# Where the second experts' row gathers stand in GpSimd's queue

## The chip, the cores and the metric

The kernel runs on one core of one Trainium2 chip. The metric is the device time of one execution in microseconds (us). The core has five engines with a queue of instructions each: TensorE (PE, with its weight loads shown apart as PEld), VectorE (DVE), ScalarE (ACT), GpSimd (POOL) and SyncE (SP). They meet only at semaphores. An engine whose next instruction waits holds up everything that is queued behind it on the same engine. Transfers run on 16 DMA engines, which serve the queues of all issuers.

## What is computed

A gated scan over 4 sequences of 5056 tokens with 256 features gives 20224 rows. These pass through a first layer of 8 experts with a fixed capacity, and then through a second layer of 8 experts, in which each row goes to the expert with the highest logit. The change touches the second layer only:

```python
logits = x @ w_gate                       # x: 20224 x 256, 8 experts
expert_idx = np.argmax(logits, axis=1)
...
for e in range(E):
    mask = expert_idx == e
    xe = x[mask]
    h = np.maximum(xe @ w1[e], 0.0)       # 256 -> 1024
    ye = h @ w2[e]                        # 1024 -> 256
    out[mask] = gate_w[mask, None] * ye
```

How many rows an expert has is known only on the chip.

## The kernel before

`scan_stage`, `route_and_experts` and `experts_top1` run one behind the other. The last of them, from about 1409 us to 2404 us of the trace, is the second layer.

**Blocks.** Rows are worked in blocks of 256, as two tiles of 128. In the profiled execution there are 83 blocks: experts 0 to 7 have 11, 7, 10, 10, 13, 13, 7 and 12 of them. The loops over an expert's blocks take their limits from `plan`, a tile in on-chip memory. Block `i` (from 0) uses the columns `i` of `rows_i` (row numbers) and `skip`.

**TensorE** (`compute(i, b)`, L1819). For each of 8 slices of 128 hidden features there is an `up` (L1804: six matmuls, 3 terms by 2 halves of the input) and a `down` (L1815: six matmuls). The `down`s follow three slices behind. After the last `up`, TensorE waits until the rows of block `i + 1` have been gathered into `xg` (L1826), transposes them (L1794, four 128x128 transposes) and then does the last three `down`s. So the transposes of block `i + 1` stand some 2.5 us ahead of the end of block `i`. There is one buffer `xg`.

**ScalarE and VectorE** turn each slice into a high part `hh` (L1851) and a low part `hl` (L1891). After the transposes ScalarE copies the last two columns of each row of `xg` to `meta` (L1855; this counts `meta_kept`). At the end of a block they scale the result by the gate: tile 0 on ScalarE (L1867), tile 1 on VectorE (L1905). These write `rows`, of which there is one buffer, once `rows_free` has been counted.

**GpSimd** has three kinds of work here, all in one queue:

- `gather(i)` (L1734 to L1745) waits until block `i - 1` has been transposed and its `meta` kept, copies two columns of row numbers to `idx` (L1739), and issues two indirect DMAs that fill `xg` with the rows of block `i` (L1743).
- `scatter_before(i)` (L1747) waits for the rows of block `i - 1` and issues two indirect DMAs that write them to the output (L1754).
- `split_up` and `split_down` (L557, L564) make the high and the low part of the next expert's two weight matrices, four casts (L549) and four subtractions (L553) each. They are done for experts 1 to 7, so in the parts of experts 0 to 6.

Turn `i` of GpSimd is `pass_on(i)`: wait until the scatter of the turn before has landed, count `rows_free`, gather block `i + 1`, scatter block `i - 1`. The turns of an expert are `first + 1` to `end`. Around the first of them stand the splits: `split_up`, turn `first + 1`, `split_down`, then the loop (L1783) over the other turns. Here `first` is the expert's first block.

**SyncE** loads the raw weights of the expert after the next (L542, L543: 1 MB each) as soon as `split_down` is done. There are seven pairs of loads (experts 1 to 7). The first stands at the beginning of the stage, and six follow a `split_down`, those in the parts of experts 0 to 5.

Of the kernel before, what the change touches and what calls it, by code (L numbers as in the profile page):

```python
# [49 lines left out]
T2 = C2 // P  # L50
# [63 lines left out]
def alone(eng, passed):  # L114

    eng.sem_inc(passed, 1)
# [440 lines left out]
def split_up(pool, c, b, split, before):  # L557

    half = F // 2
    here = [(slice(None), d, slice(q * half, (q + 1) * half)) for d in range(DH) for q in range(2)]  # L560
    split_pieces(pool, [(c.w1_raw[at], c.w1_s[b][0][at], c.w1_s[b][1][at]) for at in here], split, before)


def split_down(pool, c, b, split, before, scores=True):  # L564

    here = [(slice(None), slice(g, g + 2), slice(0, D)) for g in range(0, FC, 2)]
    split_pieces(pool, [(c.w2_raw[at], c.w2_s[b][0][at], c.w2_s[b][1][at]) for at in here], split, before)
    if scores:
        at = (slice(None), slice(None), slice(D, D + E))
        split_pieces(pool, [(c.w2g[:], c.w2_s[b][0][at], c.w2_s[b][1][at])], split, before + 2)  # L570
# [1104 lines left out]
def experts_top1(nc, c, src, w1, w2, dst):  # L1675
# [3 lines left out]
    with ExitStack() as ctx:  # L1679
# [20 lines left out]
        gathered = c.xg2_gathered  # L1700
# [16 lines left out]
        def all_blocks(eng):  # L1717
            return eng.value_load(c.plan[0:1, E - 1:E], min_val=E, max_val=B2)

        def blocks_of(eng, e):  # L1720

            end = eng.value_load(c.plan[0:1, bass.ds(e, 1)], min_val=1, max_val=B2)
            first = eng.value_load(c.plan[0:1, bass.ds(E + e, 1)], min_val=0, max_val=B2 - 1)
            return first, end

        @block.sync
        def _(sp):
            with sp.Fori(1, E) as e:
                sp.wait_ge(split, 4 * e)
                load_weights(sp, c, w1, w2, e, raw)  # L1730

        @block.gpsimd
        def _(pool):
            def gather(i):  # L1734
                pool.wait_ge(x_turned, DH * i)
                pool.wait_ge(meta_kept, i)
                pool.wait_ge(gathered, 16 * T2 * i)
                alone(pool, passed)
                pool.tensor_copy(idx[:], c.rows_i[:, bass.ds(i * T2, T2)]).then_inc(idx_ready, 1)  # L1739
                pool.wait_ge(idx_ready, i)  # L1740
                alone(pool, passed)
                for k in range(T2):
                    pool.indirect_dma_start(xg[:, k, :].bitcast(I32), None, src[:, :],  # L1743
                                            bass.IndirectOffsetOnAxis(ap=idx[:, k:k + 1].bitcast(U32), axis=0)
                                            ).then_inc(gathered, 16)  # L1745

            def scatter_before(i):  # L1747

                pool.wait_ge(rows_a, i + 1)
                pool.wait_ge(rows_b, i + 1)  # L1750
                pool.wait_ge(dest_ready, i)
                alone(pool, passed)
                for k in range(T2):
                    pool.indirect_dma_start(dst[:, :], bass.IndirectOffsetOnAxis(ap=dest[:, k:k + 1].bitcast(U32), axis=0),  # L1754
                                            rows[:, k, :], None, bounds_check=N - 1, oob_is_err=False
                                            ).then_inc(scattered, 16)

            def pass_on(i, first=False):

                if not first:  # L1760
                    pool.wait_ge(scattered, 16 * T2 * (i - 1))
                pool.sem_inc(rows_free, 1)
                gather(i + 1)
                scatter_before(i)

            pool.sem_inc(split, 4)
            gather(1)
            for e in range(E):
                first, end = blocks_of(pool, e)

                if e + 1 < E:
                    pool.wait_ge(raw, 32 * (e + 1))
                    if e > 0:
                        pool.wait_ge(h_used, FC * first + AHEAD)
                        alone(pool, passed)
                    split_up(pool, c, (e + 1) % 2, split, 4 * (e + 1))
                pass_on(first + 1, first=e == 0)
                if e + 1 < E:
                    split_down(pool, c, (e + 1) % 2, split, 4 * (e + 1) + 2, scores=False)
                second = pool.snap(first + 2, min_val=2, max_val=B2)  # L1780
                after = pool.snap(end + 1, min_val=2, max_val=B2 + 1)
                with pool.If(after > second):
                    with pool.Fori(second, after) as i:  # L1783
                        pass_on(i)
            total_blocks = all_blocks(pool)
            pool.wait_ge(gathered, 16 * T2 * (total_blocks + 2))
            pool.wait_ge(scattered, 16 * T2 * total_blocks)

        @block.tensor
# [165 lines left out]
```

## Time and profile before

| | us |
|---|---|
| median of 3 runs | 2413.83 (2413.49 to 2415.52) |
| the profiled execution, its own time | 2420.34 |
| its span in the trace | 2418.6 |
| PE busy, in the span | 2275.1 (94%) |
| POOL busy, in the span | 954.6 (39%) |
| second experts, first matmul to last | 1411.73 to about 2403.8 |

The span is what the trace covers. The 1.7 us beside it lie before and behind, and a run without the profiler was some 6.5 us shorter. TensorE is busy nearly all of the second experts' stage. GpSimd's busy time is its instructions on the engine: for an indirect DMA that is the time in which it is issued, and the data move later. "Idle before" in a row of the timeline is the time since the engine's last instruction, and behind the arrow stands what ended it.

### The profile page before, as it was taken

To read this page: it belongs to the slowest core of one execution; us is meant where nothing else is said; L and a number is where in the kernel's file an instruction comes from. 1 tells how busy PE (TensorE), PEld (TensorE's weight loads), DVE (VectorE), ACT (ScalarE), POOL (GpSimd) and SP (SyncE) were. 2 spreads that over 40 slices of the span, in tenths; PEclk is the share of its full clock that TensorE was granted. 3 is DMA by queue.
4 is the path that set the end of the run, shared out by engine and by line. 5 is a ranking of instruction groups with operands and counts; after the bars stand their busy time and mean duration, and the time that the engine had idled before them with its cause. 6 is when DMAs were issued, how large, how long until landed. Compare 5 with 4: busy or idle time off the path is not lost. (4 is left out here: it accounts for less than half of the span.)

```text
span 2418.6 us, 51799 instructions
## 1 busy us (share of the span) xinstructions
PE 2275.1 (94%) x18040; PEld 2115.4 (87%) x18041; DVE 1385.8 (57%) x3385; ACT 809.9 (33%) x2027; POOL 954.6 (39%) x1035
## 2 busy tenths in 40 slices
PE   7883699999999999999999869999999999999997
PEld 7882588888888888888898869999999999999997
DVE  8887876776767777676644443333333333333332
ACT  4440324242332423223333223333333333333332
POOL 5660133333333333333433353535353535335333
PEclk9996699999999999999999979999999999999998
DMA  7894112121211212121221131122121212111111
GB/s 271 286 318 154 53 36 71 40 68 43 71 36 40 73 39 70 44 71 36 77 75 42 45 104 46 40 82 77 43 75 47 78 44 68 53 44 42 41 45 39
DMA packets 86191, 182.95 MB, mean 76 GB/s; under 512 B 14318, under 2 KB 50929, under 8 KB 86066
## 3 DMA queue, kind: packets, MB, share of 16 engines
q0 software_dynamic: 31872, 85.58, 11.5%
q1 hardware_dynamic: 40722, 82.34, 9.9%
q10 hardware_dynamic: 13472, 13.37, 2.0%
q8 instruction: 77, 1.26, 0.2%
q14 instruction: 48, 0.39, 0.1%
HBM read 118.94 MB, written 64.13 MB: 76 GB/s over the span
## 5 line engine op out<-in xcount | busy, mean ns | idle before, releaser
L1891 DVE SCALAR_TENSOR_TENSOR m_hl<-m_hP,m_hh 128x256 fp32r<-128x256 f32 x664 | 275.0, 424 | 538.3 <-ACT m_hh L1851 486.4
L1851 ACT ACTIVATE m_hh<-m_hP 128x256 fp32r<-128x256 f32 x664 | 247.6, 384 | 516.9 <-PE m_hP L1804 516.2
L1111 ACT ACTIVATE m_hh<-m_hP 128x512 fp32r<-128x512 f32 (+1 forms) x320 | 189.9, 593 | 630.3 <-PE m_hP L976 624.6
L837 POOL DMA_INDIRECT y_rows<-spare,m_dest x164 | 180.9, 1103 | 537.9 <-DVE m_dest L1454 489.3
L1414 DVE SCALAR_TENSOR_TENSOR m_hl<-m_hP,m_hh 128x512 fp32r<-128x512 f32 (+1 forms) x320 | 218.6, 683 | 274.9 <-ACT m_hh L1111 253.2
L827 POOL DMA_INDIRECT spare<-h_rows,m_idx x164 | 193.9, 1182 | 57.1 <-issue 37.5
L1743 POOL DMA_INDIRECT xg<-y_rows,m_idx x168 | 166.0, 988 | 96.1 <-POOL m_idx L1739 70.5
L1754 POOL DMA_INDIRECT out_dram<-m_rows,m_dest x166 | 168.2, 1013 | 54.5 <-issue 54.5
L1739 POOL COPY m_idx<-rows_i 128x2 int32 (+1 forms) x84 | 15.5, 184 | 398.7 <-ACT m_meta L1855 380.9
L1804 PE MATMUL m_hP<-xh,w_0h 128*128 128x256 f32 x656 | 131.8, 282 | 11.2 <-issue 11.2
L1815 PE MATMUL m_yP<-w_1h,m_hh 128*128 128x256 f32 x672 | 139.2, 289 | 1.0 <-DVE m_hl L1891 1.0
L1804 PE MATMUL m_hP<-xh,w_1h 128*128 128x256 f32 x672 | 134.2, 281 | 2.1 <-issue 2.1
L1815 PE MATMUL m_yP<-w_0h,m_hh 128*128 128x256 f32 x656 | 136.1, 289 | 0.0
L1815 PE MATMUL m_yP<-w_1h,m_hl 128*128 128x256 f32 x672 | 134.1, 281 | 0.0
L1815 PE MATMUL m_yP<-w_1l,m_hh 128*128 128x256 f32 x672 | 133.7, 280 | 0.0
L1804 PE MATMUL m_hP<-xh,w_1l 128*128 128x256 f32 x672 | 133.3, 280 | 0.0
L1804 PE MATMUL m_hP<-xl,w_1h 128*128 128x256 f32 x672 | 133.3, 279 | 0.0
L1815 PE MATMUL m_yP<-w_0h,m_hl 128*128 128x256 f32 x656 | 131.1, 281 | 0.0
L1804 PE MATMUL m_hP<-xh,w_0l 128*128 128x256 f32 x656 | 130.9, 281 | 0.0
L1804 PE MATMUL m_hP<-xl,w_0h 128*128 128x256 f32 x656 | 130.8, 281 | 0.0
L1815 PE MATMUL m_yP<-w_0l,m_hh 128*128 128x256 f32 x656 | 130.6, 280 | 0.0
L986 PE MATMUL m_yP<-w_0h,m_hh 128*128 128x264 f32 x640 | 114.0, 300 | 4.4 <-DVE m_hl L1414 2.3
(306 smaller groups left out, 5708.7 us busy)
## 6 DMA issues: line engine op xcount, KB each, us to landing
spare<-in_moe_w_dram SPq DMA_DIRECT2D x32, 1024.0 KB, 5.6
f_in<-in_f_logit_dram SPq DMA_DIRECT2D x39, 512.0 KB, 4.5
x_in<-in_x_dram SPq DMA_DIRECT2D x39, 512.0 KB, 5.3
h_rows<-rows ACTq DMA_DIRECT2D x25, 512.0 KB, 4.5
h_rows<-spare SPq DMA_DIRECT2D x14, 512.0 KB, 6.2
xg<-y_rows,m_idx POOLq DMA_INDIRECT x168
out_dram<-m_rows,m_dest POOLq DMA_INDIRECT x166
spare<-h_rows,m_idx POOLq DMA_INDIRECT x164
```

Of the source, the lines that this page charges most:

```text
L827: pool.indirect_dma_start(xg[:, k, :], None, src[:, :], bass.IndirectOffsetOnAxis(ap=idx[:, k:k + 1].bitcast(U32), axis=0)).then_inc(gathe ...
L837: pool.indirect_dma_start(dst[:, :], bass.IndirectOffsetOnAxis(ap=dest[:, k:k + 1].bitcast(U32), axis=0), rows[(i - 1) % 2][:, k, 0:ROW].b ...
L986: mm = pe.matmul(yP[:, k, 0:WIDE], h[f % 2][:, k * P:(k + 1) * P], c.w2_s[b][s][:, f, 0:WIDE], start=(f == 0 and q == 0), stop=(f == FC - ...
L1111: act.activation(hh[f % 2][:, tokens(i)], hP[f % 2][:, tokens(i)], ACT.Relu).then_inc(hh_ready, 1)
L1414: dve.scalar_tensor_tensor(out=hl[f % 2][:, tokens(i)], in0=hP[f % 2][:, tokens(i)], scalar=0.0, in1=hh[f % 2][:, tokens(i)].bitcast(F32), ...
L1739: pool.tensor_copy(idx[:], c.rows_i[:, bass.ds(i * T2, T2)]).then_inc(idx_ready, 1)
L1743: pool.indirect_dma_start(xg[:, k, :].bitcast(I32), None, src[:, :], bass.IndirectOffsetOnAxis(ap=idx[:, k:k + 1].bitcast(U32), axis=0)).t ...
L1754: pool.indirect_dma_start(dst[:, :], bass.IndirectOffsetOnAxis(ap=dest[:, k:k + 1].bitcast(U32), axis=0), rows[:, k, :], None, bounds_chec ...
L1804: mm = pe.matmul(hP[f % AHEAD], c.w1_s[b][s][:, d, f * P:(f + 1) * P], x[:, d, :], start=(q == 0), stop=(q == len(terms) - 1))
L1815: mm = pe.matmul(yP[k], h[f % AHEAD][:, k * P:(k + 1) * P], c.w2_s[b][s][:, f, 0:D], start=(f == 0 and q == 0), stop=(f == FC - 1 and q == 2))
L1851: act.activation(hh[f % AHEAD][:], hP[f % AHEAD], ACT.Relu).then_inc(hh_ready, 1)
L1891: dve.scalar_tensor_tensor(out=hl[f % AHEAD][:], in0=hP[f % AHEAD], scalar=0.0, in1=hh[f % AHEAD][:].bitcast(F32), op0=ALU.max, op1=ALU.su ...
```

## The change

`gather(i + 1)` leaves `pass_on`. `gather(i)` now stands directly in front of `pass_on(i)` in the loop. For the first turn of each expert but expert 0 it stands ahead of `split_up`; for expert 0 that is the `gather(1)` that was there before. There is no gather of the block behind the block behind the last any more, and the wait at the end counts one gather less.

```diff
@@ -1760,7 +1760,6 @@
                 if not first:
                     pool.wait_ge(scattered, 16 * T2 * (i - 1))
                 pool.sem_inc(rows_free, 1)
-                gather(i + 1)
                 scatter_before(i)
 
             pool.sem_inc(split, 4)
@@ -1768,6 +1767,8 @@
             for e in range(E):
                 first, end = blocks_of(pool, e)
 
+                if e > 0:
+                    gather(first + 1)
                 if e + 1 < E:
                     pool.wait_ge(raw, 32 * (e + 1))
                     if e > 0:
@@ -1781,9 +1782,10 @@
                 after = pool.snap(end + 1, min_val=2, max_val=B2 + 1)
                 with pool.If(after > second):
                     with pool.Fori(second, after) as i:
+                        gather(i)
                         pass_on(i)
             total_blocks = all_blocks(pool)
-            pool.wait_ge(gathered, 16 * T2 * (total_blocks + 2))
+            pool.wait_ge(gathered, 16 * T2 * (total_blocks + 1))
             pool.wait_ge(scattered, 16 * T2 * total_blocks)
```

GpSimd's queue at an expert with splits, from the subtractions of `split_up` to those of `split_down`. `w_0h` and `w_0l` are the parts of the weights (the first pair those of w1, the second those of w2), `xg` is what a gather fills, `out_dram` what a scatter writes:

```order
 L553 TENSOR_TENSOR w_0l<-spare,w_0h 128x512 x4
 L1761 REGISTER_ALU
-L1735 ISA
-L1737 REGISTER_ALU
-L1739 ISA
-L1739 COPY m_idx<-rows_i 128x2
-L1743 DMA xg<-y_rows,m_idx 128x258 x2
-L1751 REGISTER_ALU
+L1749 REGISTER_ALU
 L1754 DMA out_dram<-m_rows,m_dest 20224x256 x2
 L549 CAST w_0h<-spare 128x2x256 x4
 L553 TENSOR_TENSOR w_0l<-spare,w_0h 128x2x256 x4
```

The gather between the two splits is gone. It was the gather of block `first + 2`.

GpSimd's loop over an expert's other turns, before:

```order
190 L1783 ISA
191 L1735 ISA
192 L1737 REGISTER_ALU
193 L1739 ISA
194 L1739 COPY m_idx<-rows_i 128x2
195 L1743 DMA xg<-y_rows,m_idx 128x258 x2
196 L1754 DMA out_dram<-m_rows,m_dest 20224x256 x2
```

and the same loop in the changed kernel, with the two splits' last instruction in front of it:

```order
182 L553 TENSOR_TENSOR w_1l<-spare,w_1h 128x2x256 x4
183 L1783 REGISTER_ALU
184 L1783 COMPARE_AND_BRANCH
185 L1784 UNCONDITIONAL_BRANCH
186 L1784 ISA
187 L1737 REGISTER_ALU
188 L1739 ISA
189 L1739 COPY m_idx<-rows_i 128x2
190 L1743 DMA xg<-y_rows,m_idx 128x258 x2
191 L1761 ISA
192 L1749 REGISTER_ALU
193 L1754 DMA out_dram<-m_rows,m_dest 20224x256 x2
```

The loop holds the same copy and the same four DMAs in the same order, but the gather in it is that of the turn's own block, one block earlier in the count. The first gather of the loop, that of block `first + 2`, now stands behind `split_down`. The orders of TensorE and SyncE are the same in both kernels.

## Rows read from the trace of the kernel before

**Rows 1.** Waits of 1380 to 2418 us: us in total, times, longest

```profile
PE m_tP L1794 <- DMA xg<-y_rows,m_idx: 3.0, 2, 2.1
```

**Rows 2.** Timeline of one ordinary turn: start us, us, engine, line, what

```profile
1506.69 0.46 PEld L1794 LDWEIGHTS m_tP<-ident,xg 128*128 128x128 f32 x4
...
1507.84 0.18 POOL L1739 COPY m_idx<-rows_i 128x2 int32 x1 [5.82 <-ACT m_meta L1855]
...
1508.86 1.01 POOL L1743 DMA_INDIRECT xg<-y_rows,m_idx  x1 [0.83 <-POOL m_idx L1739]
...
1509.58 0.48 DVE L1905 TENSOR_SCALAR m_rows<-m_yP,m_gate 128x256 f32<-128x256 f32 x1 [0.99 <-PE m_yP L1815]
...
1510.17 0.97 POOL L1743 DMA_INDIRECT xg<-y_rows,m_idx  x1 [0.30 <-DVE m_rows L1905]
...
1511.45 1.01 POOL L1754 DMA_INDIRECT out_dram<-m_rows,m_dest  x1 [0.30 <-issue]
...
1512.77 1.01 POOL L1754 DMA_INDIRECT out_dram<-m_rows,m_dest  x1 [0.30 <-issue]
...
1518.45 0.46 PEld L1794 LDWEIGHTS m_tP<-ident,xg 128*128 128x128 f32 x4
```

**Rows 3.** Timeline of the first experts: a scatter's DMA behind the wait it had

```profile
723.25 0.16 DVE L1454 TENSOR_TENSOR m_dest<-m_dest_f,m_skip 128x4 int32<-128x4 f32 x1
...
724.32 1.01 POOL L837 DMA_INDIRECT y_rows<-spare,m_dest  x1 [11.66 <-DVE m_dest L1454]
```

**Rows 4.** Timeline: block 0's gather, alone, and the transposes that waited for it

```profile
1399.12 1.18 POOL L858 DMA_INDIRECT xg<-y_rows,rows_i  x1 [0.30 <-issue]
...
1402.13 0.29 PEld L1077 LDWEIGHTS m_tP<-ident,xg 128*128 128x128 f32 x2 [14.19 <-issue]
```

**Rows 5.** Timeline of POOL around the start of expert 1

```profile
1549.04 2.30 POOL L549 CAST w_0h<-spare 128x512 fp32r<-128x512 f32 x4
1551.42 5.04 POOL L553 TENSOR_TENSOR w_0l<-spare,w_0h 128x512 fp32r<-128x512 f32 x4
1556.41 0.18 POOL L1739 COPY m_idx<-rows_i 128x2 int32 x1
...
1558.73 0.96 POOL L1743 DMA_INDIRECT xg<-y_rows,m_idx  x1 [0.31 <-DVE m_rows L1905]
```

**Rows 6.** Timeline of PE around the same start: transposes of blocks 11, 12 and 13

```profile
1542.07 0.60 PE L1794 MATMUL m_tP<-ident,xg 128*128 128x128 f32 x4
1545.35 0.50 PE L1804 MATMUL m_hP<-xh,w_1h 128*128 128x256 f32 x2 [0.55 <-issue]
...
1555.16 0.60 PE L1794 MATMUL m_tP<-ident,xg 128*128 128x128 f32 x4
1567.07 0.60 PE L1794 MATMUL m_tP<-ident,xg 128*128 128x128 f32 x4
```

**Rows 7.** Timeline: two gathers beside a weight load, and the transposes that waited

```profile
1439.25 0.37 SPq L542 DMA_DIRECT2D spare<-in_moe_w_dram  x1
...
1441.37 0.96 POOL L1743 DMA_INDIRECT xg<-y_rows,m_idx  x1 [0.30 <-issue]
...
1447.83 0.66 PE L1794 MATMUL m_tP<-ident,xg 128*128 128x128 f32 x4 [0.88 <-DMA xg<-y_rows,m_idx]
...
1777.47 0.96 POOL L1743 DMA_INDIRECT xg<-y_rows,m_idx  x1 [0.30 <-issue]
...
1783.48 0.66 PE L1794 MATMUL m_tP<-ident,xg 128*128 128x128 f32 x4 [2.12 <-DMA xg<-y_rows,m_idx]
```

**Rows 8.** Timeline of PE: block 0 of the stage, from its first matmul

```profile
1411.73 0.79 PE L1804 MATMUL m_hP<-xh,w_0h 128*128 128x256 f32 x2 [8.48 <-issue]
...
1423.09 0.60 PE L1794 MATMUL m_tP<-ident,xg 128*128 128x128 f32 x4
```

**Rows 9.** Stretches: us, busy of PE, PEld, DVE, ACT, POOL, granted clock, DMA share, GB/s

```profile
1416.00:1416.50 0.50, 0.50 (x4) 0.50 (x4) 0.11 (x1) 0.36 (x1) 0.00 (x0) 0.58 1.01 326
...
2406.00:2406.50 0.50, 0.00 (x0) 0.00 (x0) 0.00 (x0) 0.00 (x0) 0.50 (x1) 0.79 0.35 91
```

## The prediction

> **What bounds the kernel now.** I read the summary by engine first (TensorE busy 94% of the span), then the waits, then the timelines of an ordinary turn and of an expert's start. From 1411.7 to 2403.8 us the second experts are a row of TensorE blocks, one every 11.76 us (the two weight loads of the transposes in [rows 2]). GpSimd is not what TensorE waits for: for a gather TensorE waited twice, 3.0 us in all [rows 1]. The reader is to see the reason in [rows 2]: the gather goes out as soon as the single buffer `xg` is free (1507.84), its second DMA starts at 1510.17, and the transposes that need it come at 1518.45. That is 8.28 us from the DMA's start to the need. The change gives this slack away, since each gather now goes behind the scatter of the block before. So the question is how long a gather needs from the moment at which the rows of a finished block are ready.
>
> **Ordinary turns.** After the change GpSimd waits for `rows`, scatters, then gathers for the transposes that end the running block. The chain is, from one start of the transposes:
> - 3.37 us until `rows` is ready (1506.69 to 1509.58 + 0.48) [rows 2]
> - 0.91 us from the semaphore to the first scatter DMA. This wait is not in the second stage, where the scatter always stands behind a running gather; the nearest row is the first experts' scatter, 723.41 to 724.32 [rows 3]
> - 1.32 us to the second scatter DMA, 1.01 us for it, 1.02 us from the copy of the indices to the first gather DMA, 1.31 us to the second [rows 2]
> - from its start to the data: 3.01 us in [rows 4], where the DMA itself took 1.18 instead of 0.97 us; I take 2.80.
>
> Together 11.74 us against 11.76 us. The wait for the former scatter, which now stands behind the gather, costs nothing: that scatter was issued two DMAs earlier, and `rows` is wanted only at the end of the block. So ordinary turns are level to a few hundredths, and I can't say from the rows on which side. Of the 82 gathers that the change moves (blocks 2 to 83, with 83 read by no `up`), 7 are the late ones of the next part and 7 stand ahead of a split or at the start of expert 7, where TensorE itself loses time between experts (13.09 us between the transposes at 1542.07 and 1555.16 [rows 6]), so 68 remain. I take 0.05 us each, 3.4 us, with the bounds 0 (every link 0.1 shorter) and 0.3 each, 20 us.
>
> **The first turns of experts 0 to 6.** Here is the main cost. The gather of block `first + 2` stood between the two splits and now stands behind `split_down`. A split takes 7.42 us (1549.04 to 1556.46 [rows 5]); `split_down` has as many casts and subtractions of the same size, and I take the same for it. For expert 1:
> - transposes of block `first` at 1542.0, `rows` ready at 1545.3, scatter DMAs at 1546.2 and 1547.5, copy of indices 1548.5, gather of `first + 1` at 1549.5 and 1550.9. It lands at 1553.7, ahead of the transposes at 1555.1 [rows 6]: no wait.
> - `split_up` 1551.8 to 1559.2. It is now behind that gather. The rows of block `first` are ready at 1555.1 + 3.4 = 1558.5, so the scatter is not held by them and follows at 1559.5 and 1560.9.
> - `split_down` 1561.8 to 1569.2, the copy at 1569.2, the gather DMAs at 1570.3 and 1571.6. Before, the second one was at 1558.73 [rows 5].
> - Alone it lands 2.80 us later, at 1574.4, against transposes that were due at 1567.0 [rows 6]: TensorE waits 7.4 us.
> - It is not alone. SyncE loads 2 MB of weights as soon as `split_down` ends. In the kernel before, the loop's first gather met the same load in the same order, the load 2.1 us ahead of the second gather DMA: 1439.25 and 1441.37, and the transposes could start only at 1447.8 [rows 7]. That is 6.4 us from the DMA's start instead of 2.8. At the other late gather it was 5.9 us (1777.47 to 1783.4 [rows 7]). I take 6.15, between them. The wait is then 10.7 us.
>
> The six loads that follow a `split_down` belong to experts 0 to 5, expert 6 has none behind it. Expert 0's first part begins with weights that come late, but its two splits and gathers stand in the same row; I count it the same. So 6 x 10.7 + 7.4 = 71.6 us. The gathers that waited before, 0.88 and 2.12 us [rows 7], now follow a long stop and a full block, so their 3.0 us go: net 68.6 us. Bounds: with no collision 6 x 3.3 = 20 us less; with 6.4 us in each 1.5 us more.
>
> The Trainium skill has a rule against this collision: by "DMA: Bandwidth & Descriptors", section "Queues, rings and completion order", each DMA engine takes turns between the queues that have work, packet by packet. By that rule a gather of a few packets an engine would hardly notice the load, and the sum would be 20 us less. [Rows 7] speak against it, with 6.4 us.
>
> **TensorE's clock.** The granted clock was at the lower of its two levels (0.50, 1.2 GHz) while the stage began, and rose to 2.4 GHz at about 1416.4 us [rows 9], 4.7 us after the first matmul at 1411.73 [rows 8]. At the end of the kernel it fell some 2.5 us after TensorE stopped (0.79 in the half microsecond from 2406.0) [rows 9]. All seven waits of this forecast are longer than that, so each should be followed by slow matmuls. Price: 4.7 us at half speed lose 2.35 us; block 0 took 11.36 us from its first matmul to the transposes [rows 8], another expert's first block 9.81 us (1545.35 to 1555.16 [rows 6]), which is 1.55 us. I take 2.1 between them: 7 x 2.1 = 14.7 us, bounds 0 and 16.5 us. These blocks give GpSimd more time, so no further gather is late for it.
>
> **The rest.** The last turn no longer issues a gather ahead of its scatter. Before, the first scatter DMA came 1.39 us behind `rows` (1510.06 to 1511.45 [rows 2]); now 0.91. That is 0.5 us off the end. One gather less moves 264 KB less, hidden. The last expert has no splits, so its first turns are ordinary.
>
> **Sum.** 68.6 + 14.7 + 3.4 - 0.5 = 86.2 us on the profiled execution, whose own time is 2420.34: 2506.5. The median of the runs shown is 2413.83, 6.5 us below that execution; the added waits don't depend on this, so the forecast is 2413.8 + 86.2 = 2500 us, 3.6% slower.
>
> **Rivals.**
> - *The gather beside the weight load lands as if alone.* The time is 20 us less: 2480. For it: only two such gathers were seen waiting. Against it: both were late. The rule of the Trainium skill named above ("DMA: Bandwidth & Descriptors") would give this one. Chance 0.13.
> - *Ordinary turns are late too.* If the chain is 12.0 to 12.2 us instead of 11.74, TensorE waits in each of 68 turns and the period of the stage becomes the chain: 14 to 31 us more beyond my 3.4 at most, 2511 to 2528. For it: the sum has no slack, and its two uncertain links (0.91 and 2.80) come from other stages. Chance 0.17.
> - *The clock doesn't fall.* 14.7 us less, 2486. For it: the rows show the clock fall only once TensorE has stopped for good. Against it: that fall came sooner after the stop than any of the seven waits would end. Chance 0.06.
> - *Not slower.* GpSimd would issue the gather's DMAs while its casts and subtractions run, so that `split_down` holds up nothing. Then the seven waits are not there, and the 3.0 and 0.5 us are gained: 2410, within 0.2% of before. It decides from the point at which the gather of `first + 2` starts its second DMA by 1567.0 - 2.8 = 1564.2 instead of 1571.6. Against it: the copy of the indices behind a split starts where the split ends (1556.41 [rows 5]), though nothing held it back, and a scatter's DMA starts 0.30 us behind a gather's [rows 2]. Chance 0.04.
> - The forecast as summed: chance 0.60, own range 2490 to 2512.
>
> **Numbers.** The range 2474 to 2522 takes in the forecast, the clock and the collision rivals and half of the late ordinary turns. A measurement of this kernel can tell about 0.2% (4.8 us) from no change. Slower by over 0.2%: 0.96. Within 0.2%: 0.03, nearly all of the last rival. Faster by over 0.2%: 0.01.
>
> **What would show it.** In the changed kernel the waits of the transposes (L1794) for the gather should be about 75 us, in seven waits of 7 to 11 us, one an expert but the last, the one without a weight load the shortest; ahead of each, on GpSimd, two splits with only a scatter between them. Behind each the granted clock should be 0.50 for 4 to 5 us. In ordinary turns the second gather DMA should start some 2.8 us ahead of the transposes, and the period be 11.8. If the period is 12 or more, the second rival holds. If the seven waits are all near 7.4 us, the first does. If there are none, my reading of GpSimd's queue is wrong.

## The result, and the profile after

| | before | after |
|---|---|---|
| median of 5 runs, us | 2413.49 (2412.79 to 2415.52) | 2506.16 (2504.57 to 2508.11) |
| ratio to before, with its 95% interval | | 1.0383 (1.0371 to 1.0395) |
| the profiled execution, its own time | 2420.34 | 2504.57 |
| its span | 2418.6 | 2502.8 |

The change costs 92.7 us. The forecast was 2500 in a range of 2474 to 2522.

The page of after, its parts 1 and 5 (in the last: what is done, how often, busy us and mean ns, then the idle time before it and what ended that):

```profile
PE 2283.4 (91%) x18040; PEld 2123.6 (85%) x18041; DVE 1390.1 (56%) x3385; ACT 820.0 (33%) x2027; POOL 953.0 (38%) x1032
...
L1796 PE MATMUL m_tP<-ident,xg 128*128 128x128 f32 x332 | 54.7, 290 | 79.8 <-DMA xg<-y_rows,m_idx 79.7
```

TensorE does the same work (18040 matmuls in both; 2275.1 us busy before, 2283.4 now, and the 8 us more fit the stretches at the lower clock further down), but 79.7 us of idle time stand in front of the transposes, and a gather ended them. The lines have moved: what was L1794 is L1796, L1905 is L1907. The waits of 1380 to 2503 us (in total, times, longest) answer to [rows 1], where it was 3.0 us in two waits:

```profile
POOL out_dram L1754 <- DVE m_rows L1907: 503.0, 76, 11.8
...
PEld m_tP L1796 <- DMA xg<-y_rows,m_idx: 83.4, 18, 12.2
...
PE m_tP L1796 <- DMA xg<-y_rows,m_idx: 79.7, 15, 12.0
```

The first line is the new wait of GpSimd, in nearly every turn: it now stands in front of the scatter, with the gather queued behind it. That costs nothing by itself. An ordinary turn of after, answering to [rows 2]:

```profile
1507.05 0.48 DVE L1907 TENSOR_SCALAR m_rows<-m_yP,m_gate 128x256 f32<-128x256 f32 x1 [0.99 <-PE m_yP L1817]
...
1508.46 1.01 POOL L1754 DMA_INDIRECT out_dram<-m_rows,m_dest  x1 [6.10 <-DVE m_rows L1907]
1509.77 0.99 POOL L1754 DMA_INDIRECT out_dram<-m_rows,m_dest  x1 [0.30 <-issue]
...
1511.80 1.01 POOL L1743 DMA_INDIRECT xg<-y_rows,m_idx  x1 [0.83 <-POOL m_idx L1739]
...
1513.12 0.96 POOL L1743 DMA_INDIRECT xg<-y_rows,m_idx  x1 [0.30 <-issue]
...
1515.90 0.46 PEld L1796 LDWEIGHTS m_tP<-ident,xg 128*128 128x128 f32 x4
```

The reader is to see that the last line has no bracket, so TensorE didn't wait, and that the second gather DMA starts 2.78 us ahead of it instead of 8.28. The slack is spent. From `rows` ready (1507.53) to the scatter's DMA are 0.93 us.

GpSimd at the start of expert 1, answering to [rows 5], with the weight load of SyncE (`SPq`) and the transposes of block `first + 2`:

```profile
1564.15 5.02 POOL L553 TENSOR_TENSOR w_0l<-spare,w_0h 128x512 fp32r<-128x512 f32 x4
...
1569.33 1.02 POOL L1754 DMA_INDIRECT out_dram<-m_rows,m_dest  x1 [0.17 <-issue]
...
1570.66 1.01 POOL L1754 DMA_INDIRECT out_dram<-m_rows,m_dest  x1 [0.31 <-issue]
...
1571.65 2.30 POOL L549 CAST w_0h<-spare 128x512 fp32r<-128x512 f32 x4
...
1574.03 4.98 POOL L553 TENSOR_TENSOR w_0l<-spare,w_0h 128x512 fp32r<-128x512 f32 x4
...
1578.97 0.17 POOL L1739 COPY m_idx<-rows_i 128x2 int32 x1
...
1579.18 0.37 SPq L542 DMA_DIRECT2D spare<-in_moe_w_dram  x1
...
1581.30 0.96 POOL L1743 DMA_INDIRECT xg<-y_rows,m_idx  x1 [0.30 <-issue]
...
1587.32 1.12 PE L1796 MATMUL m_tP<-ident,xg 128*128 128x128 f32 x4 [10.90 <-DMA xg<-y_rows,m_idx]
```

Between the two splits is only a scatter. The gather goes out behind `split_down`, in step with the load, and the transposes start 6.0 us after its second DMA. Stretches around that wait (us, busy time of PE, PEld, DVE, ACT and POOL, granted clock, DMA share, GB/s):

```profile
1576.00:1581.00 5.00, 0.42 (x4) 0.22 (x2) 0.42 (x1) 0.38 (x1) 4.14 (x5) 1.00 0.13 19
...
1582.00:1587.00 5.00, 0.00 (x0) 0.00 (x0) 0.00 (x0) 0.00 (x0) 0.26 (x1) 0.50 1.04 373
...
1587.00:1587.50 0.50, 0.18 (x1) 0.18 (x2) 0.00 (x0) 0.11 (x1) 0.00 (x0) 0.50 0.26 78
...
1588.00:1591.00 3.00, 3.00 (x16) 3.00 (x15) 0.92 (x3) 0.74 (x2) 0.00 (x0) 0.50 0.03 5
...
1592.00:1593.00 1.00, 1.00 (x11) 1.00 (x10) 0.48 (x1) 0.68 (x2) 0.00 (x0) 1.00 0.00 0
```

TensorE stops at 1576.4. The clock is still full up to 1581 and falls behind that, during the stop. It stays at its lower level of 1.2 GHz for some 4 us of work behind it (16 matmuls in 3 us, later 11 in one), and comes back at 1591 to 1592. The DMA engines are full until 1587.1, and the transposes start 0.2 us later: the gather was there about when the last of the load was.

**Where the time is.** I took the distance from one block's transposes to the next one's, for all 82 pairs of both traces, by the start of the transposes' weight loads, and grouped them by the block that the later transposes are for (an expert's blocks counted from `first`):

| distances ending at | before | after | difference |
|---|---|---|---|
| block `first + 2`, 7 of them | 83.28 | 157.53 | +74.25 |
| block `first + 3`, 7 | 86.53 | 94.83 | +8.30 |
| block `first + 1` of experts 1 to 7, 7 | 90.44 | 89.85 | -0.59 |
| the other 61 | 717.69 | 723.02 | +5.33 |
| sum | 977.94 | 1065.23 | +87.3 |

The table gives 87.3 us and the medians 92.7. The stage began 2.4 us earlier in after's profiled execution (1409.31 instead of 1411.73) and ended 0.7 us earlier behind its last rows, so that the two profiled executions differ by 84.2 us. The one of before was 6.9 us above the median of its runs, that of after 1.6 us below its own. In which stage before's profiled execution spent those 6.9 us the record doesn't show, so the place of what the table leaves open isn't known either. The profiler by itself doesn't make an execution so much longer: the profiled executions of the other kernels are 1.6 us below to 4.5 us above their medians. Beside the experiments below the kernel before had medians of 2414.78, 2419.72 and 2419.29 us, on three chips. On the second of these a repeat of after cost 88.8 us (ratio 1.0362), and the distances in its trace sum to 1068.4 us.

### The profile page after: what moved, and what is told of

Read it like the earlier page. It is cut to its first block and busy times, and to the rows that moved or that the text cites. A ratio compares the mean times of both kernels' runs of the same rounds, so it can differ in the third digit from the quotient of the medians.

```text
span 2502.8 us, 51866 instructions
## 1 busy us (share of the span) xinstructions
PE 2283.4 (91%) x18040; PEld 2123.6 (85%) x18041; DVE 1390.1 (56%) x3385; ACT 820.0 (33%) x2027; POOL 953.0 (38%) x1032
## 3 DMA queue, kind: packets, MB, share of 16 engines
q0 software_dynamic: 31776, 85.32, 10.9%
## 5 line engine op out<-in xcount | busy, mean ns | idle before, releaser
L1893 DVE SCALAR_TENSOR_TENSOR m_hl<-m_hP,m_hh 128x256 fp32r<-128x256 f32 x664 | 282.1, 425 | 524.4 <-ACT m_hh L1853 524.4
L1853 ACT ACTIVATE m_hh<-m_hP 128x256 fp32r<-128x256 f32 x664 | 254.8, 384 | 502.4 <-PE m_hP L1806 502.4
L1806 PE MATMUL m_hP<-xh,w_0h 128*128 128x256 f32 x656 | 131.8, 282 | 11.3 <-issue 11.3
L1796 PE MATMUL m_tP<-ident,xg 128*128 128x128 f32 x332 | 54.7, 290 | 79.8 <-DMA xg<-y_rows,m_idx 79.7
```

What stands on the lines that cost most here:

```text
L1796: t = pe.transpose(tP[d][:, k * P:(k + 1) * P], xg[:, k, d * P:(d + 1) * P], c.ident[:])
L1806: mm = pe.matmul(hP[f % AHEAD], c.w1_s[b][s][:, d, f * P:(f + 1) * P], x[:, d, :], start=(q == 0), stop=(q == len(terms) - 1))
L1853: act.activation(hh[f % AHEAD][:], hP[f % AHEAD], ACT.Relu).then_inc(hh_ready, 1)
L1893: dve.scalar_tensor_tensor(out=hl[f % AHEAD][:], in0=hP[f % AHEAD], scalar=0.0, in1=hh[f % AHEAD][:].bitcast(F32), op0=ALU.max, op1=ALU.su ...
```

## The experiments

**My theory.** Three things make up the change's cost: the seven gathers that now stand behind `split_down`, the clock that falls while TensorE waits for them, and a landing that the weight load puts off. **The rivals**: that ordinary turns cost a good part of it (the chain through the scatter has no slack), that the load only happens to be beside the gather, and that the clock is a sign and no cost. Experts here have at least 7 blocks, which the edits make use of. Each experiment was run beside the kernel before. The ratios below are to it.

### One part alone: only the first turns

The kernel before, with only the gather of block `first + 2` moved behind `split_down`. Ordinary turns stay as they were.

```diff
-                gather(i + 1)
+                if ahead:
+                    gather(i + 1)
                 scatter_before(i)
...
-                pass_on(first + 1, first=e == 0)
+                pass_on(first + 1, first=e == 0, ahead=e + 1 == E)
                 if e + 1 < E:
                     split_down(pool, c, (e + 1) % 2, split, 4 * (e + 1) + 2, scores=False)
+                    gather(first + 2)
```

> The kernel before, but for experts 0 to 6 the gather of block first + 2 is moved behind split_down; all other gathers stay ahead of the scatter of the turn before theirs. Theory: seven waits of 7 to 12 us and seven slow blocks come with it, the short waits of ordinary turns don't: 2413.5 + 73.7 - 3.0 + 12.8 = 2497, within 2492 to 2501. Rival, that the long waits need the later gathers in front of them as well (the gather of first + 1, and split_up behind it): the waits are shorter by the 2.3 us by which split_up starts sooner, 7 x 2.3 = 16 us less, 2481.

Measured: 2494.20 us (2493.43 to 2498.54), ratio 1.0326 (1.0309 to 1.0343), 79.4 us over before. Its waits:

```profile
PEld m_tP L1796 <- DMA xg<-y_rows,m_idx: 73.4, 7, 11.1
```

They are seven: six of 10.9 to 11.1 us and one of 7.3. The short waits of after are absent. The distances to `first + 2` and `first + 3` are 155.86 and 97.18 us, together 83.2 more than before, and the other 68 are 3.9 us shorter in all than before's, for which I have no reason. So 79 of the 93 us come with this one gather an expert. The move of the others is worth the rest, some 14 us by the ratios (their intervals leave it between 9 and 19), of which the two spans show 6 (2502.8 and 2496.8) and the distances 7.9 (1065.23 and 1057.32). Which is nearest I can't say.

### The load out of the way

After, but SyncE's load waits until the late gather has landed. GpSimd waits for that landing too, ahead of the turn's scatter.

```diff
                 sp.wait_ge(split, 4 * e)
+                sp.wait_ge(load_ok, e)
                 load_weights(sp, c, w1, w2, e, raw)
...
+                if e + 1 < E:
+                    gather(second)
+                    pool.wait_ge(gathered, 16 * T2 * (second + 1))
+                    pool.sem_inc(load_ok, 1)
+                    pass_on(second)
```

> The changed kernel, but SyncE's weight load that follows split_down waits in addition until the gather of block first + 2 has landed. Theory: the load is what makes six of the seven gathers land 3.3 us later than alone, so the six waits of 10.6 to 12.0 us become about 7.4 us like the seventh: 2506.2 - 6 x 3.4 = 2486, within 2482 to 2490. Rival, that the gathers are late by themselves and the load has no share: 2506. If the DMA engines took turns packet by packet between the two queues, as the rule of the Trainium skill says (DMA: Bandwidth & Descriptors, Queues, rings and completion order), the change would also be small.

Measured: 2485.20 us (2484.57 to 2485.65), ratio 1.0289 (1.0272 to 1.0306). The same place as above, in expert 1:

```profile
1579.07 0.96 POOL L1745 DMA_INDIRECT xg<-y_rows,m_idx  x1 [0.30 <-issue]
...
1581.81 1.12 PE L1805 MATMUL m_tP<-ident,xg 128*128 128x128 f32 x4 [7.71 <-DMA xg<-y_rows,m_idx]
1582.02 0.37 SPq L542 DMA_DIRECT2D spare<-in_moe_w_dram  x1
```

2.74 us from the DMA's start to the transposes instead of 6.02, and the load follows. All seven waits (of the weight loads) are 7.4 to 8.8 us. The distances to `first + 2` fall by 20.6 us (157.53 to 136.97), and nothing else changes by more than 0.7. The load costs six gathers 3.4 us each: it is the cause, and not merely beside them. After itself agrees. Its seventh late gather, of expert 6, has no load, and the transposes start 2.9 us after its second DMA, where the other six took 5.7 to 6.4 us.

### The clock kept up

After, with 84 matmuls into the transposes' PSUM tile ahead of the long wait. Nothing reads their result. They take most of the time of the wait.

```diff
...
+                if busy is not None:
+                    with pe.If(busy < E - 1):
+                        for _ in range(84):
+                            pe.matmul(tP[0], c.w1_s[b][0][:, 0, 0:P], xh[:, 0, :], start=True, stop=True)
                 pe.wait_ge(gathered, 16 * T2 * (i + 2))
...
```

> The changed kernel, but TensorE does 84 matmuls more, whose result nobody reads, ahead of its wait for the gather of block first + 2 in experts 0 to 6 (84 x 0.117 = 9.8 us). Theory: the slow blocks behind the long waits (12.8 us together beyond ordinary ones) come from the clock, which fell to 1.2 GHz while TensorE stood still; with TensorE busy it stays up, and the matmuls are hidden in the waits but for 2.4 us in expert 6, whose wait is 7.4 us: 2506.2 - 12.8 + 2.4 = 2496, within 2493 to 2499. Rival, that these blocks are slow for another reason (the chain through GpSimd): 2506.2 + 2.4 = 2509.

Measured: 2495.81 us (2493.89 to 2497.22), ratio 1.0331 (1.0314 to 1.0348). The 84 matmuls, the transposes behind them, and the stretch that follows:

```profile
1574.68 9.96 PE L1831 MATMUL m_tP<-xh,w_1h 128*128 128x256 f32 x84
...
1586.08 0.66 PE L1796 MATMUL m_tP<-ident,xg 128*128 128x128 f32 x4 [1.45 <-DMA xg<-y_rows,m_idx]
...
1586.00:1590.00 4.00, 3.92 (x34) 3.92 (x35) 1.31 (x4) 1.70 (x5) 0.00 (x0) 1.00 0.00 0
```

The gather is as late as in after, but the clock is 1.00 behind the wait, with 34 matmuls in 4 us. The distances to `first + 3` come to 83.54 us instead of 94.83. 11.3 us are the clock's. With useless work for TensorE the kernel is 10 us faster than with a wait (medians 2495.81 and 2506.16, though not run side by side). In the distances to `first + 2` the extra matmuls cost 3.9 us.

### The gather back between scatter and split

After, but the gather of `first + 2` goes out ahead of `split_down` again, as before.

```diff
                 if e + 1 < E:
+                    gather(first + 2)
                     split_down(pool, c, (e + 1) % 2, split, 4 * (e + 1) + 2, scores=False)
...
+                if e + 1 < E:
+                    pass_on(second)
```

> The changed kernel, but for experts 0 to 6 the gather of block first + 2 is put between the scatter of turn first + 1 and split_down, and the loop begins with that turn's scatter. All other gathers stay where the change put them. Theory of the forecast: the seven long waits (73.7 us in the changed kernel) and the slow clock behind each of them (7 blocks that took 12.8 us longer than ordinary ones) hang on split_down alone, so both go; the gather's second DMA starts about 2.8 us ahead of the need and no weight load is near it. 2506.2 - 73.7 - 12.8 = 2420, within 2416 to 2425. Rival, that each gather behind its scatter costs, in all turns: it stays above 2440.

Measured: 2452.86 us (2450.28 to 2453.70), ratio 1.0153 (1.0136 to 1.0170). I was wrong. The time is where my rival put it (above 2440), but its reason isn't the one, for the loss isn't in all turns. The transposes for `first + 2` hardly wait any more (four times, 0.2 to 1.1 us), but those for `first + 3` do:

```profile
1573.99 1.03 POOL L1754 DMA_INDIRECT out_dram<-m_rows,m_dest  x1
1574.01 0.37 SPq L542 DMA_DIRECT2D spare<-in_moe_w_dram  x1
...
1578.69 0.97 POOL L1743 DMA_INDIRECT xg<-y_rows,m_idx  x1 [0.30 <-issue]
...
1583.70 0.72 PEld L1800 LDWEIGHTS m_tP<-ident,xg 128*128 128x128 f32 x4 [3.65 <-DMA xg<-y_rows,m_idx]
```

`split_down` now holds up the scatter of the next turn, the gather of `first + 3` stands behind that scatter, and both meet the load. By distances: 85.88 us to `first + 2`, 105.91 to `first + 3`, 91.65 to `first + 4`. In the last the clock is at work, which had fallen in six waits of 3.4 to 3.6 us. The other distances are within 0.8 us of after's in all. What follows: the split isn't harmful only in front of the one gather. With no gather a block ahead, `split_down` makes one late at either of the two places tried. The distances to `first + 2`, `first + 3` and `first + 4` are together 82 us longer than before's where it stands ahead of the gather, and 31 us where it stands behind.

### Both: the gather back, and the load behind

The kernel above, and SyncE's load waits until the gather of `first + 3` has landed.

```diff
...
+                    with pool.Fori(third, fourth) as i:
+                        gather(i)
+                        pool.wait_ge(gathered, 16 * T2 * (i + 1))
+                        pool.sem_inc(load_ok, 1)
+                        pass_on(i)
...
```

> The kernel of the run early_again (gather of first + 2 ahead of split_down), but the weight load waits until the gather of block first + 3 has landed. In early_again that gather followed split_down and a scatter and was beside the load: its second DMA started at 1578.69 and the transposes came at 1583.70, 3.65 us after TensorE was ready. Theory: alone it lands 2.8 us after its start, at 1581.5, so the six waits are 1.4 instead of 3.6 to 3.8 us, too short for the clock to fall: 6 x 2.2 = 13 us less for the waits and 9 us less for the clock: 2452.9 - 22 = 2431, within 2425 to 2436. Rival, that the load has no share: 2453.

Measured: 2434.14 us (2433.71 to 2435.65), ratio 1.0056 (1.0041 to 1.0072). The distances to `first + 3` are 92.91 us instead of 105.91, those to `first + 4` 82.26 instead of 91.65. In the first of the two a wait is left:

```profile
1582.69 0.42 PEld L1810 LDWEIGHTS m_tP<-ident,xg 128*128 128x128 f32 x4 [1.47 <-DMA xg<-y_rows,m_idx]
```

Of the 93 us of the change all but 14 are gone. By distances 15 are left over before: 6.4 to `first + 3` (92.91 against 86.53), 2.7 to `first + 2`, and 6.8 in the 61 others, where after has 5.3. All gathers but the seven that went back still stand as in after.

### A longer step in every turn

After, with a fill of a 128x512 tile on GpSimd ahead of each gather of the loop. Nothing reads the tile. It is there to see how much slack ordinary turns have.

```diff
                     with pool.Fori(second, after) as i:
+                        pool.memset(step[:], 0.0)
                         gather(i)
```

> The changed kernel, with one more instruction of GpSimd (a fill of 128x512 numbers that nobody reads, an estimate of 0.3 to 0.6 us by the casts of that size, 0.58 us each) ahead of each gather of the loop. Theory: ordinary turns are level, so what a gather starts later TensorE waits longer: 68 turns x 0.3 to 0.6 = 20 to 41 us more than the changed kernel, and nearly every ordinary turn shows a wait. Rival, that ordinary turns still have slack of half a microsecond or more, since the profile shows only 8 short waits: less than 8 us more.

Measured: 2540.06 us (2539.13 to 2541.01), ratio 1.0497 (1.0481 to 1.0513). That is 31.6 us over a repeat of after (below), whose kernel before ran at 2419.72 on its chip, against 2419.29 here.

```profile
PEld m_tP L1798 <- DMA xg<-y_rows,m_idx: 120.1, 74, 12.5
...
1502.53 0.56 POOL L1786 MEMSET m_step<- 128x512 f32 x1
1503.00 0.21 POOL L1740 COPY m_idx<-rows_i 128x2 int32 x1
...
1520.33 0.42 PEld L1798 LDWEIGHTS m_tP<-ident,xg 128*128 128x128 f32 x4 [0.47 <-DMA xg<-y_rows,m_idx]
```

The copy starts 0.47 us later than in after, and the gather is waited for in nearly all turns (74 waits, 18 in after). The period is 12.1 to 12.2 us. In the 54 distances that end at neither `first + 1` nor `first + 2`, `+ 3` or `+ 4` the sum is 666.71 us where after has 640.72, 0.48 a turn. So all of the added 0.47 shows: ordinary turns of after have no slack that I can measure, and they lose nothing by it as long as nothing is added.

### The eight short waits

Beside the seven long waits after has eight of 0.3 to 1.7 us, 6.0 us in all, by the matmuls of the transposes. (Their weight loads show eleven, each 0.2 us longer; the three more are at last blocks of experts too.) Five of the eight are at the last block of an expert and one at the block behind the last of all. In these, places without a row all point at the same row of zeros (the last block of expert 7 has 27 rows for its 256 places). Two are elsewhere. The gather of expert 7's last block in after:

```profile
2469.53 0.97 POOL L1743 DMA_INDIRECT xg<-y_rows,m_idx  x1 [0.30 <-issue]
...
2473.14 0.42 PEld L1796 LDWEIGHTS m_tP<-ident,xg 128*128 128x128 f32 x4 [0.79 <-DMA xg<-y_rows,m_idx]
```

3.6 us from the second DMA to the transposes instead of 2.8. At the eight last blocks it is 3.0 to 3.3 us with fewer than 100 empty places (four blocks) and 3.6 to 3.7 us with more (four), and 3.8 at the block behind the last, in which all 256 are empty. The experiment keeps 128 rows of zeros, one for each partition, and lets the empty place in partition `p` read row `p` of them. The kernel is otherwise after.

```diff
-            sp.dma_start(dst[E * N:E * N + 1, :], zero[:]).then_inc(zero_stored, 16)
+            sp.dma_start(dst[E * N:E * N + P, :], zero[:]).then_inc(zero_stored, 16)
...
-                st.do(dve.tensor_scalar(c.rows_i[:, tiles], row_f[:, tiles], float(E * N), None, ALU.add))
+                st.do(dve.tensor_scalar(c.rows_i[:, tiles], row_f[:, tiles], pad[:], None, ALU.add))
```

> The changed kernel, but the empty places of a block don't all read the one zero row behind the data: place p reads a zero row p of its own (128 zero rows instead of one). The changed kernel's short waits for a gather (8 in all, 6.0 us) are, but for two, those of experts' last blocks and of the block behind the last, and in those rows most places are empty. Theory: many reads of one row make such a gather 0.6 to 1.0 us slower, and with its own rows each such wait goes: six waits, 3.5 us less, 2502.7 if the changed kernel is at 2506.2 on this chip. Rival, that these gathers are slow by chance or by the block's place: no change (within 1 us).

Measured: 2503.86 us (2503.20 to 2505.49), ratio 1.0346 (1.0332 to 1.0360). A repeat of after on the same chip:

> The changed kernel itself, beside the next ones on the same chip: 2506, within 2503 to 2509.

Measured: 2508.51 us (2506.82 to 2509.69), ratio 1.0362 (1.0348 to 1.0376). The own rows are 4.65 us faster, with ranges that don't meet. The waits of the repeat, then those of the experiment and its gather of the same block:

```profile
PEld m_tP L1796 <- DMA xg<-y_rows,m_idx: 85.3, 18, 12.2
```

```profile
PEld m_tP L1798 <- DMA xg<-y_rows,m_idx: 79.0, 9, 12.2
...
2482.34 0.96 POOL L1745 DMA_INDIRECT xg<-y_rows,m_idx  x1 [0.30 <-issue]
...
2485.17 0.42 PEld L1798 LDWEIGHTS m_tP<-ident,xg 128*128 128x128 f32 x4
```

2.83 us again, and no wait. All last blocks are at 2.8 to 2.9 us. The two waits that are not at last blocks are still there (1.13 and 1.88 us by the weight loads, 1.04 and 1.84 in after). These two gathers don't land late (2.8 us in after), they go out late. Between their two DMAs GpSimd stands still for 2.20 us instead of 0.30. The second of them in after, and what stands at the same place of the count before:

```profile
2164.43 0.96 POOL L1743 DMA_INDIRECT xg<-y_rows,m_idx  x1 [2.20 <-issue]
```

```profile
2089.22 1.01 POOL L1754 DMA_INDIRECT out_dram<-m_rows,m_dest  x1 [2.27 <-issue]
```

In all twelve traces it is the 444th and the 556th indirect DMA of GpSimd that come so late. In before both are a scatter's second DMA, and no transposes wait for such a scatter itself. (But the first of them stands ahead of expert 3's `split_up`, and expert 3 has the longer of the two waits of [rows 1], 2.12 us, where experts 1, 2, 4 and 5 have none.) After has two DMAs fewer ahead of each scatter, so the same place in the count falls on the second DMA of a gather without slack. What happens at that place the record doesn't show. Expert 3's long wait, 12.02 us where the other five with a load have 10.6 to 11.0, fits it too: the first of the two late DMAs stands ahead of its `split_up`, which starts 1.8 us later behind the transposes of `first` than expert 1's.

### Before, with the load out of the way

The two waits of [rows 1] stand beside a load too. So: the kernel before, where the load waits until the loop's first gather has landed. GpSimd makes that wait, ahead of its scatter.

```diff
...
+                        gather(i + 1)
+                        pool.wait_ge(gathered, 16 * T2 * (i + 2))
+                        pool.sem_inc(load_ok, 1)
+                        scatter_before(i)
...
```

> The kernel before with one thing of the lesson: SyncE's weight load waits until the loop's first gather has landed. Theory: the two waits for a gather beside a weight load (0.88 and 2.12 us) go, nothing else moves: 3.0 us less than before, 2410.5 to 2411.5 if before is at 2413.5 to 2414.8. Rival, that the load, now some 4 us later, meets the next scatter and holds rows_free: no gain or up to 5 us more.

Measured: 2432.02 us (2430.98 to 2436.49), ratio 1.0047 (1.0033 to 1.0061): slower than before by 12.3 us. So the rival had the right mechanism, and even it gave the loss only up to 5 us. The waits for gathers did go (the distances to `first + 3` are 82.09 us, 86.53 before), but those to `first + 4` went from 82.83 to 104.33:

```profile
1443.44 0.37 SPq L542 DMA_DIRECT2D spare<-in_moe_w_dram  x1
...
1445.61 1.01 POOL L1756 DMA_INDIRECT out_dram<-m_rows,m_dest  x1 [0.30 <-issue]
...
1452.71 0.16 DVE L1912 TENSOR_TENSOR m_dest<-m_meta,skip 128x2 int32 x1 [5.10 <-POOLq L1764]
...
1453.04 0.18 POOL L1741 COPY m_idx<-rows_i 128x2 int32 x1 [6.42 <-DMA out_dram<-m_rows,m_dest]
...
1454.04 0.79 PE L1828 MATMUL m_yP<-w_0h,m_hh 128*128 128x256 f32 x2 [3.32 <-DVE m_hl L1904]
```

The load now meets the scatter. That scatter's landing frees `rows`, and what waits for it went on 7.1 us after its last DMA had started (1445.61 to 1452.71). VectorE stood behind `rows_free` for 5.1 us, and with it the `hl` that TensorE wanted.

### Before, with the load a turn later

Neither a gather nor a scatter that is wanted soon should stand beside the load. In the kernel before I let SyncE load at the start of the loop's second turn, when the scatter of the first has landed.

```diff
...
+                    with pool.Fori(third, fourth) as i:
+                        pool.wait_ge(scattered, 16 * T2 * (i - 1))
+                        pool.sem_inc(load_ok, 1)
+                        pool.sem_inc(rows_free, 1)
+                        gather(i + 1)
+                        scatter_before(i)
...
```

> The kernel before, with the weight load held until the scatter of the loop's first turn has landed, which is the start of the loop's second turn. In before_load_behind the load took the two waits for gathers away (block first + 3 came 4.4 us sooner in all) but met that scatter, and rows_free came up to 6 us late. Theory: here the load meets only a gather that is on time and has 8.3 us, and a scatter whose successor is wanted late: 3.0 us less than before, ratio 0.9988. Rival, that any scatter beside the load holds up the next block's hand-over: slower than before by 5 us or more, as in before_load_behind.

Measured: 2416.52 us (2415.49 to 2417.31) against 2419.29 for before beside it, ratio 0.9988 (0.9979 to 0.9997), from 11 and 15 runs. No transposes of the stage wait for a gather any more. Its ratio is the lowest of all these kernels. The interval leaves out 1, but 0.12% is less than the 0.2% that the forecast took as what a measurement can tell.

```profile
1443.16 1.01 POOL L1756 DMA_INDIRECT out_dram<-m_rows,m_dest  x1 [0.30 <-issue]
1445.86 0.37 SPq L542 DMA_DIRECT2D spare<-in_moe_w_dram  x1
...
1447.02 0.18 POOL L1741 COPY m_idx<-rows_i 128x2 int32 x1 [2.85 <-ACT m_meta L1870]
```

The load goes out when the scatter's data have gone, and the next gather, whose copy is here at 1447.02, is wanted only a block later.

## Why the prediction was right, point by point

- **The seven late gathers, 71.6 us: right.** They are where the forecast puts them, and measured 10.77, 10.90, 10.96, 12.02, 10.97, 10.62 and 7.44 us, 73.7 in all, 2.1 us more than forecast. The shortest is expert 6's, the one without a load behind its split. With that one gather moved in the kernel before they came to 72.0 (73.4 by the weight loads).
- **The collision, 3.35 us each by [rows 7]: right.** Taking the load away gave 20.6 us back for six. (By [rows 7] the second gather took 6.0 us and not 5.9, so the value between the two is 6.2, and the sum 0.5 us more.) So the step that chose the row over the rule of the page holds. By the round robin of the Trainium skill ("DMA: Bandwidth & Descriptors", section "Queues, rings and completion order"), packet by packet, a gather should hardly be held by a load. It has 96 packets here, by which the counts of the two profiles differ with one gather less. The same section of the Trainium skill says that a semaphore's write lands only after every earlier write of that DMA engine, across its queues. That fits what the windows show, a gather that is known to have landed about when the load has, but no run here tells it apart from turns that are merely shared unevenly.
- **The clock, 14.7 us: right in kind, a little too large in after.** In the distances to `first + 3` after has 12.6 us over its ordinary 11.74, 1.8 us a wait where I took 2.1. Keeping the clock up gave 11.3 us back. (In the kernel with only the first turns moved it was 2.1 each.) The term was mis-sized by 2 us.
- **The 3.0 us of old waits that go: right.** No transposes for `first + 3` wait in after. Before, these distances were 4.2 us over ordinary ones (86.53 against 7 x 11.76 = 82.3), so a little more than the 3.0 went.
- **Ordinary turns, 3.4 us: the size about right, the form wrong.** I spread 0.05 us over 68 turns. Most turns lose nothing at all (11.65 to 11.80 us from transposes to transposes, 11.73 in the mean, and 11.76 before), and eight late gathers lose 6.0 us. The chain of 11.74 us was right to a few hundredths, as the added step shows. The step that failed is that all gathers go out and land alike: I took one price, 2.80 us, and the last blocks of experts pay 3.0 to 3.7. Two other gathers had their second DMA 2.20 us behind the first instead of 0.30.
- **The end, 0.5 us: right.** Rows ready to scatter took 0.93 us (2489.17 to 2490.10), forecast 0.91, before 1.43.
- **From the trace to the runs.** The sum of 86.2 us stands against 87.3 in the stage, 84.2 between the two profiled executions, 92.7 between the medians and 88.8 with the repeat. The 6 us by which the forecast is low against the medians come in with the step from before's profiled execution to its runs, 6.9 us, while after's differ by only 1.6 the other way. I had said that the added waits don't depend on those 6.9 us. The record neither shows nor refutes that.
- **Luck.** That the sum is within 1.1 us of the table owes something to errors that cancel: 2.1 us too little for the late gathers and 2.0 us too much for the clock.
- **The rivals.** No collision: excluded by the experiment with the load behind. Ordinary turns late: not in after but for the eight, but 0.47 us more on GpSimd brings it on. (Its price was added up wrong. A chain of 12.0 to 12.2 us is 18 to 31 us over 11.74 in 68 turns, and less the 3.4 in the sum that gives 2514 to 2528, not 2511 to 2528.) A clock that doesn't fall and a split that holds nothing up: excluded by after's trace.

Where I was wrong was in two of the expectations, and both times for one reason: I moved one queued piece away from a split or a load, and didn't ask what stands there then. With the gather back ahead of `split_down` it was the next scatter and the gather behind it. With the load behind the gather it was the scatter.

## What to carry to other kernels

Here the gather issued one block ahead is what hid every irregular piece of work in its queue. Before giving that distance away, list what stands in the queue or beside it only once in a while (here a 7.4 us split, a 2 MB load and a pause of 2.2 us between two DMAs), not only what stands there in every turn. When the matrix engine waits, count its slow matmuls behind the wait as well, which here came to a sixth of the wait itself. When you move a transfer out of another's way, look at what it stands beside at its new place and who waits for that.

## What the runs showed of the hardware that I had not expected

- A small gather beside a 2 MB load is known to have landed about when the load has. In after the DMA share falls at 1587.1 and the transposes start at 1587.32; at the other five such places they start between 0.2 us ahead of the fall and 0.6 us behind it. In the kernel with the gather back between scatter and split it was 1.0 us behind (1582.7 and 1583.70). A scatter beside the load took 7.1 us from its last DMA's start to what waited for it. In the kernel with the load a turn later, where the load itself waits for a scatter, it was 2.7 us (1443.16 to 1445.86).
- Gathers in which many places name one and the same row land 0.2 to 1.0 us later (3.0 to 3.8 instead of 2.8 us from the second DMA's start). Spreading those places over 128 rows removed it and gave 4.65 us in the whole.
- In all twelve traces GpSimd stood idle for 2.2 to 2.4 us ahead of its 444th and its 556th indirect DMA, where 0.30 us stand between the two DMAs of other gathers and scatters. What that DMA belongs to depends on the order of issue.
- The granted clock fell in stops of only some 3.5 us: in the kernel with the gather back between scatter and split the weight load of the transposes behind such a stop took 0.72 us instead of 0.42, and the clock was 0.56 in the mean of the 3 us that followed.

```profile
1580.00:1583.00 3.00, 0.25 (x3) 0.05 (x1) 0.42 (x1) 0.38 (x1) 0.00 (x0) 1.00 0.96 346
1584.00:1587.00 3.00, 3.00 (x17) 3.00 (x16) 0.92 (x3) 0.75 (x2) 0.00 (x0) 0.56 0.02 5
```
